# Linear attention with two MLP mixers on one core: other places for late VectorE, ScalarE and GpSimd work at the end of the first phase

## What is computed

```python
state = alpha[:, :, t, :, None] * state + einsum('bhd,bhe->bhde', k[:, :, t], v[:, :, t])
y[:, :, t] = einsum('bhd,bhde->bhe', q[:, :, t], state)
```

```python
h = xt @ U @ V            # xt is x turned; rank 32
u = x + h.transpose(0, 2, 1)
x = u + np.maximum(u @ w_ch1, 0) @ w_ch2
```

## Time and profile before

| | |
|---|---|
| median of 3 runs | 748.88 us |
| the profiled execution, its own time | 749.1 us |
| its span (first to last instruction) | 747.3 us |
| mean granted TensorE clock | 1.000 |
| PE busy | 716.0 us, 96% of the span |
| DVE busy | 347.7 us, 47% |
| ACT busy | 327.8 us, 44% |
| POOL busy | 202.0 us, 27% |

### The profile page before, as it was taken

How to read it: one execution, slowest core, us unless ns; L and a number is a source line. 1 busy time by engine, 2 the same in 40 slices (tenths; PEclk the granted TensorE clock), 3 DMA queues, 4 the chain that set the end, 5 groups by cost and what they waited for, 6 DMA issues and landing times.

```text
span 747.3 us, 25682 instructions
## 1 busy us (share of the span) xinstructions
PE 716.0 (96%) x11408; PEld 676.9 (91%) x11408; DVE 347.7 (47%) x612; ACT 327.8 (44%) x570; POOL 202.0 (27%) x142
## 2 busy tenths in 40 slices
PE   2798899999999999999999999999999999999998
PEld 2688798899998999999999899999999998999998
DVE  6888664645654644764552412115315323431531
ACT  5787546444636445536434322225134232432412
POOL 5504480310450310350220422231330250132031
PEclk9999999999999999999999999999999999999999
DMA  9415401320401220401000332140021002001001
GB/s 359 153 46 174 147 9 39 120 65 14 151 6 41 83 85 31 151 3 46 34 4 3 96 127 63 54 153 6 1 71 58 1 33 95 0 0 63 0 0 63
DMA packets 16076, 49.48 MB, mean 66 GB/s; under 512 B 1680, under 2 KB 8080, under 8 KB 15472
## 3 DMA queue, kind: packets, MB, share of 16 engines
q1 hardware_dynamic: 15984, 48.09, 18.5%
HBM read 38.65 MB, written 9.44 MB: 64 GB/s over the span
## 4 chain that ended last, share of the span: by engine, by line
PE 91%; DVE 3%; issue 1%; ACT 1%; DVEq 0%
PE HB L836 26%; PE ZB L836 9%; PE ZB L913 7%; PE ZB L915 7%; PE ZB L914 7%; PE SB L836 6%; PE SB L713 4%; PE ZB L949 3%; PE HB L949 3%; PE SB L818 2%; PE SB L949 2%; PE SB L827 2%; PE HB L954 2%; PE ZB L954 2%; PE SB L773 2%; PE SB L954 1%
## 5 line engine op out<-in xcount | busy, mean ns | idle before, releaser
L1436 DVE SCALAR_TENSOR_TENSOR hid_lo<-HB,hid_hi 128x384 fp32r<-128x384 f32 x96 | 53.3, 556 | 142.8 <-ACT hid_hi L1141 141.9
L1141 ACT ACTIVATE hid_hi<-HB 128x384 fp32r<-128x384 f32 x96 | 47.2, 492 | 157.6 <-PE HB L836 157.5
L836 PE MATMUL HB<-uh,w1h 128*128 128x384 f32 x288 | 103.0, 358 | 2.5 <-DVE ul L1432 1.5
L913 PE MATMUL ZB<-hid_hi,w2h 128*128 128x384 f32 x288 | 98.6, 342 | 0.0
L836 PE MATMUL HB<-ul,w1h 128*128 128x384 f32 x288 | 96.7, 336 | 0.0
L915 PE MATMUL ZB<-hid_lo,w2h 128*128 128x384 f32 x288 | 96.6, 335 | 0.0
L836 PE MATMUL HB<-uh,w1l 128*128 128x384 f32 x288 | 96.4, 335 | 0.0
L914 PE MATMUL ZB<-hid_hi,w2l 128*128 128x384 f32 x288 | 96.2, 334 | 0.0
L666 POOL TENSOR_TENSOR gl<-gated,gh 128x384 fp32r<-128x384 f32 x32 | 32.5, 1015 | 179.6 <-ACT gh L1156 179.6
L996 ACT COPY Qd<-Q 48x768 f32<-48x768 f32 x84 | 73.1, 870 | 13.9 <-PE SB L713 5.5
L626 POOL TENSOR_TENSOR Q<-Q,bk 112x768 f32<-112x768 f32 x13 | 24.7, 1904 | 174.4 <-ACT Qd L996 174.4
(11 more groups left out here) (232 smaller groups left out, 1476.8 us busy)
## 6 DMA issues: line engine op xcount, KB each, us to landing
Q<-in_q SPq DMA_DIRECT2D x8, 768.0 KB, 5.8
AL<-in_al SPq DMA_DIRECT2D x7, 768.0 KB, 4.4
K<-in_k SPq DMA_DIRECT2D x7, 768.0 KB, 4.2
Vt<-in_v SPq DMA_DIRECT2D x8, 576.0 KB, 3.7
mid<-x2s SPq DMA_DIRECT2D x8, 576.0 KB, 4.3
x<-mid SPq DMA_DIRECT2D x4, 1152.0 KB, 6.0
out<-o_sb SPq DMA_DIRECT2D x24, 192.0 KB, 1.8
x2s<-in_w SPq DMA_DIRECT2D x9, 384.0 KB, 4.0
```

The source lines that it names most:

```text
L836: last = nc.tensor.matmul(dst, weights(x, w), moving(y, m), start=(n == 0 and x == y == 0), stop=(n == total - 1 and y == 1))
L913: nc.tensor.matmul(bank, w2h[:, i, cols], hi, start=(i == 0), stop=False)
L1141: nc.scalar.activation(hid_hi[:, i % HID, :], HB[i % 2][:, 0:TILE], ACT.Relu).then_inc(h_hi, 1)
L1436: nc.vector.scalar_tensor_tensor(hid_lo[:, i % HID, :], HB[i % 2][:, 0:TILE], 0.0, hid_hi[:, i % HID, :].bitcast(F32), ALU.max, ALU.subtra ...
```

## The change

Five edits at the end of the first phase and the start of the second:

1. DVE's square copies of group 0 (Ad into A, L1402) move behind group 0's last key scaling, those of group 1 behind group 0's key copies.
2. V's three split parts move behind group 1's KV step and the low parts of pieces 0 to 2.
3. `att_start(1, 0)`, the seven decay products, moves ahead of the units "xu" and "u" on DVE.
4. The low parts of pieces 3 to 5 move from DVE to POOL, which begins with them once the seven products are done.
5. On ACT the two copies of the level 1 queries of (1, 0) no longer follow those of level 0: one stands behind hid_hi of h0, the other behind hid_hi of h1.

```diff
@@ module level
-LOW1 = {(1, KV_STEP): [0, 1, 2, 3], (1, AV_STEP + 1): [4], (1, AV_STEP + 2): [5]}
-SPLIT_V = {(1, LEVELS - 1): [0], (0, T_STEP): [1], (1, KV_STEP): [2]}
@@ gpsimd, split_low and the main list
-                pool.wait_ge(w_hi, n + 1 - STAGE)
+                pool.wait_ge(w_hi, n + 1 if n < W1_PIECES else n + 1 - STAGE)
...
-            pool.wait_ge(w_lo, W1_PIECES)
+            pool.wait_ge(tot_ready[0], 2 * (LEVELS - 1))
+            pool.wait_ge(w_lo, STAGE)
+            for n in range(STAGE, W1_PIECES):
+                split_low(n)
@@ scalar, spread and att_second take the parts to copy
-            def att_second(a, g):
+            def att_second(a, g, parts=range(2)):
...
                         att_start(1, 0, False)
-                        att_second(1, 0)
+                    if b == 0 and kind == "h" and i < 2:
+                        att_second(1, 0, [i])
@@ vector, first phase
-                if (g, n) == (1, MASKED):
-                    for h in range(GROUPS):
-                        square_copies(h, QUARTERS[2:])
+                if (g, n) == (0, LEVELS - 1):
+                    square_copies(0, QUARTERS[2:])
                 if (g, n) == (0, T_STEP):
                     key_copies(g)
+                    square_copies(1, QUARTERS[2:])
                 if n == KV_STEP:
                     first_queries(g, LEVELS - 1)
-                for m in LOW1.get((g, n), []):
-                    split_low(m)
-                for part in SPLIT_V.get((g, n), []):
-                    split_v(part)
+            for m in range(STAGE):
+                split_low(m)
+            for part in range(3):
+                split_v(part)
+            att_start(1, 0)
...
                     low(b, kind, i)
-                    if b == 0 and (kind, i) == ("u", NU - 1):
-                        att_start(1, 0)
```

More of the change, by code:

```diff
@@ L991, in _, with spread @@
         def _(act):
-            def spread(a, g, n, first):
-                for hh in range(2):
+            def spread(a, g, n, first, parts=range(2)):
+                for hh in parts:
                     r = slice(hh * ROW1, hh * ROW1 + HD)
@@ L1017, in att_second @@
                     act.wait_ge(zeroed_q[0], 2)
-                spread(a, g, 1, False)
+                spread(a, g, 1, False, parts)
             def first_spread(g, n):
```

## The result

| | before | after |
|---|---|---|
| median | 748.88 us (747.95 to 748.99, 5 runs) | 754.43 us (752.63 to 755.65, 5 runs) |
| the profiled execution, its own time | 749.1 us | 753.9 us |
| its span | 747.3 us | 752.1 us |
| mean granted TensorE clock | 1.000 | 0.989 |
| PE busy | 716.0 us | 715.2 us |

A forecast was written before the change was run, and what follows sets the result against it. PE was taken as the bound, so delays before 85 us are not made up. Terms +0.5, +1.0 and +1.8 gave 3.3 us: span 747.3 to 750.6, profiled time 752.4, median 752.2; range 749.0 to 755.2.

The forecast's parts named there:

- the sum: Delay at the scores of level 1: +0.5, +1.0 and +1.8 us, together 3.3 us.
- the rival with the lower clock: TensorE slows in the gap before level 1's scores: 2.4 us more, 5.7 in all, 754.6 us; chance 0.25.
- the likeliest case: DVE and POOL take turns before level 1's scores and the clock is kept: 752.2 us; chance 0.34.
- Edit 1, -0.18: End of the first phase: K ready without the square copies in front, transposes 0.18 us earlier; bounds 0 and -0.46.
- V's split and the products, 0: DVE after 58.91 us: products end at 66.6, no cost from later low parts; bounds 0 and +0.4 us.
- The second copy, +0.5: ACT's last level 1 copy waits for h1, so DVE's query product starts at 76.5, scores 0.5 us later.
- the 76 that was to be a sign of a wrong forecast: The first query product on DVE starting before 76 us, not at 76.5, would show the forecast wrong.
- h2's gain: h2 starts on PE at 75.0 instead of 76.19, 1.1 us gained, which ends at level 1's scores.
- Turns at the port, +1.0 and +1.8: POOL's pieces alternate with DVE's query products and K's scaling before level 1: 1.0 us, then 1.8 us more.
- Clock kept: TensorE keeps full clock through the gap before level 1's scores; with turns, chance 0.34.
- pieces of PE behind it with the same lengths: Expected sign: behind level 1's scores at 82.9 us, PE's pieces last as long as before.
- The same work later behind it: Behind level 1's scores the same work comes in the same order, only later by the 3.3 us.

The follow-up runs named there:

- e7: Kernel before the change with only ACT's two level 1 query copies moved behind hid_hi of h0 and h1; 749.99 us, ratio 1.0016 to before.
- e8: Changed kernel with DVE making both level 1 query copies, POOL's pieces between its scalings, (1, 1)'s query and value loads earlier; 749.79 us, ratio 1.0008 to before.
- e9: Changed kernel with POOL splitting only 32 of 768 columns of pieces 7 and 8, part of the result left out; 752.53 us, ratio 1.0034 to before.
- e1: Changed kernel with 24 unneeded matmuls put on PE between h2 and the scores of level 1; 760.29 us, ratio 1.0143 to before.
- e10: Changed kernel with each pair of POOL's sums into x2s one query scaling later; 755.24 us, ratio 1.0087 to before.
- e2: Changed kernel with both level 1 query copies put back right behind those of level 0 on ACT; 753.34 us, ratio 1.0053 to before.
- e3_pieces_behind: Changed kernel with POOL's splits of pieces 7 and 8 behind its first two query scalings, low parts of 9 to 11 one later; 757.17 us, ratio 1.0122.
- e4: Changed kernel with POOL's pieces 7 and 8 moved behind and the level 1 query copies put back early; 751.77 us, ratio 1.0033 to before.
- e6: e4 with (1, 1)'s query and value loads ahead of pieces 9 to 11, piece 11's low part right behind piece 10's; 750.67 us, ratio 1.0034 to before.

## Why the prediction was right, and where it was not

The forecast said slower, and it is slower, by 5.55 us where the sum had 3.3. The range holds 754.43 only because it took in the rival with the lower clock; the likeliest case, 752.2 with the clock kept, is not what happened.

- **Edit 1, -0.18.** The transposes start 5.32 us behind the scores of level 7, and 5.41 before: -0.09. L802 stands as far behind them as before. Right in sign and without weight.
- **V's split and the products, 0.** The products end at 66.2, POOL's first w1l follows at 66.28, and h2 starts without a wait. PE's wait before L882 grew from 0.51 to 0.78 us, and the next one, before h0, fell from 0.76 to 0.60. Right.
- **The second copy, +0.5.** e7 measures +0.74, and the +0.5 is +0.68 without the -0.18 in it: right. The query product starts 4.29 us behind the scores of level 0, and 4.27 were forecast. At 75.99 it is by 0.01 us under the 76 that was to be a sign of a wrong forecast, but only because this whole trace is 0.71 us early at level 0. The statement that h2's gain ends at level 1 is right too: e8 shows the gain at 1.16 us when the copies are early.
- **Turns at the port, +1.0 and +1.8.** The order was as forecast: subtraction, first product, cast, second product, subtraction, K. The rows say +0.92 for the first product (1.87 - 0.95), 0.62 for the second and 0.78 for K: 2.32 in place of 2.8, and e9 gives 2.33. In sum, from level 0 to level 1, 3.08 us against 3.5 (the 3.3 of the sum and the 0.18 that were to be won ahead of level 0). But the reading of the earlier trace rows that led to turns was wrong: there DVE asks 0.05 us after POOL's scaling has started, and POOL's next instruction goes ahead of it too, so POOL does keep what it holds over two instructions. Behind level 0 the turns came out all the same; at level 5 POOL went ahead twice in a row, as in those rows.
- **Clock kept: wrong.** This step of the likeliest case failed: "pieces of PE behind it with the same lengths". The rival (0.25) is what happened. Its price in the profiled execution was 1.3 us by e1, not 2.4; but e10, with the same lists up to this place and a gap of 5.90 us, paid 2.72, so 2.4 lies inside what the runs show. The argument against it, that gaps of 0.98 and 1.59 us did no harm, was true and did not bear on a gap of 6 us. Six kernels whose last gap was 2.51 us or more had a level 1 to 2 of 5.6 to 7.0 us, the six with 1.57 to 1.66 us had 4.27 to 4.30. All of PE's idle time between the two scores sorts the twelve in the same way (3.3 us or more, 2.6 or less), so the runs don't say which of the two counts. The Trainium skill warns of idle gaps between bursts ("TensorE: Matmul & The Clock Gate", section "Why this matters for your kernels"). The twelve traces agree that a long gap halves the clock; e7's 2.51 us is shorter than the gap that its table names, and there the measurement decides.
- **The same work later behind it: wrong.** The forecast moved everything behind level 1 in one block. DVE and POOL are released there by different events (scores, Qd copies, pieces), so their overlaps changed, and the scaling of level 5 went from 2.30 to 3.20 us and asked in a worse moment: +1.58 us from level 5 to level 6, +1.3 from level 2 to the transposes.

So the rival's 754.6 is close to 754.43 partly by luck: in the profiled execution its clock was 1.1 us too dear, and 1.3 us elsewhere was missing. The start of a run varies by more than either: 42.95 and 41.62 for the same instruction.

## What to carry to other kernels

Before you move GpSimd work, list every DVE instruction with two SBUF inputs that it may come to lie beside, all the way to where the queues meet again, and price each at the rest of GpSimd's instruction, and at two or three more of them where GpSimd has them ready (3.20, 5.00 and 5.13 us in place of 0.95); one moved piece shifts the meetings of all later ones. A wait saved on PE is worth nothing if the next instruction waits for something that was not made earlier: two gaps that become one longer gap also put the clock at risk. Compare intervals between instructions that both kernels have, not starts.

## What the runs showed of the hardware

- The granted clock fell to 0.50 (1.2 of 2.4 GHz) in or behind gaps of 2.51 to 5.90 us and not behind 1.57 to 1.66 us; in the low stretch matmuls of 384 columns follow each other every 0.32 us, at full clock every 0.17. Read in stretches of 1 us, it fell about 2.3 us into the gap in after, and in e2 and e7 only 1.6 to 1.7 us behind the gap's end, with PE at work again.
- The price went with the work that PE did in the low stretch and not with the gap. It is 0.41 to 0.46 of that time in all six:

| kernel | last gap, us | PE's work at the low clock, us | level 1 to 2 above 4.27, us |
|---|---|---|---|
| after | 5.88 | 3.2 | 1.32 |
| e2_copies_first | 3.72 | 3.4 | 1.58 |
| e7_before_copies_late | 2.51 | 3.4 | 1.57 |
| e9_short_pieces | 3.52 | 5.2 | 2.24 |
| e3_pieces_behind | 3.52 | 5.3 | 2.25 |
| e10_sums_late | 5.90 | 6.3 | 2.72 |

- Who gets in when both wait is not settled by who asked first. In the kernel before, K's scaling of level 5 asked 0.40 us into a POOL subtraction and ran ahead of the two sums behind it (2.30 us in all); after, it asked 1.38 us into the same subtraction and both sums, whose rows start later than its own, ran first (3.20 us). The Trainium skill's "SBUF — State Buffer", section "Who interferes with whom", lets the order of issue decide; the first case agrees; the second doesn't, as far as a row's start tells when an instruction was issued, and nor does, of the kernel before. What decides between the two is open. In e4 DVE waited for three POOL instructions, of which two started after it had asked.
- A POOL cast with one input is in these turns like a subtraction: 1.56 us beside DVE's product, 0.82 alone.
- A copy of the queries into Qd takes DVE about as long as ACT (1.97 us for two in e8, 1.8 on ACT).
- Some stops of PE in the midst of equal matmuls end 2.2 to 2.9 us behind a packet of the DMA queue "q8 instruction". One is in all twelve traces at about 41 us, after 57 of the 96 matmuls of level 6 of group 1 in the first phase (0.69 to 1.33 us), ahead of everything that was changed and with no load under way.
- The transposes at the end of the first phase took 2.13 us in most kernels, and 1.18 us in e6, e9 and e10. The granted clock from 44 to 50 us reads as follows in before, after and e6:

```profile
44.00:50.00 6.00, 5.98 (x81) 5.79 (x78) 5.60 (x10) 5.02 (x11) 0.00 (x0) 1.00 0.01 3
44.00:50.00 6.00, 6.00 (x75) 5.88 (x72) 4.80 (x8) 4.28 (x10) 0.00 (x0) 0.50 0.01 3
44.00:50.00 6.00, 5.94 (x96) 5.62 (x92) 4.77 (x8) 5.29 (x12) 0.00 (x0) 1.00 0.01 3
```

  The same work at the two speeds under a record of 1.00 says that this record alone doesn't prove the full clock.
